# GpSimd takes three of seven taps of the second piece, and two engines' early work is reordered

## The reference

```python
w = exp(weight_gen - max(weight_gen, axis=-1))        # (4, 4096, 8, 7)
w = w / (sum(w, axis=-1) + 1e-9)
out = einsum('bshk,bskhg->bshg', w, x_unf)            # 7 taps over time, 8 heads of 24 channels
x = out.reshape(16384, 192)
h = x @ w_in                                          # 192 -> 2048
g = h * (1.0 / (1.0 + exp(-1.702 * h)))
return g @ w_out                                      # 2048 -> 192
```

## Time and profile before

| | |
|---|---|
| median of 3 runs | 1128.45 us (1128.18 to 1128.71) |
| profiled execution, its own time | 1128.58 us |
| its span, first to last instruction | 1126.8 us |
| PE busy | 1111.8 us (99%), 9748 matmuls |
| PEld busy | 914.2 us (81%) |
| DVE busy | 801.0 us (71%) |
| ACT busy | 622.1 us (55%) |
| POOL busy | 10.5 us (1%), 11 instructions |
| chain that ended last | PE 97%, ACT 1%, DVE 1% |
| granted TensorE clock | 0.999 of full speed |

### The profile page before, as it was taken

One profiled execution on the slowest core, in us unless ns is written; L12 is line 12 of the kernel. 1 busy time (PEld: TensorE's weight loads), 2 busy tenths in 40 slices (PEclk: granted clock), 3 DMA queues, 4 the chain that ended last, 5 costly groups with the idle time before them and its releaser, 6 DMA issues.

```text
span 1126.8 us, 21690 instructions
## 1 busy us (share of the span) xinstructions
PE 1111.8 (99%) x9748; PEld 914.2 (81%) x9748; DVE 801.0 (71%) x709; ACT 622.1 (55%) x659; POOL 10.5 (1%) x11
## 2 busy tenths in 40 slices
PE   6999999999999999999999999999999999999998
PEld 4788888888888888888888888888888888888886
DVE  7999988587685866859668496785957768586322
ACT  6767655555544656455464555645555555454543
POOL 2000000000000000000000000000000000000000
PEclk9999999999999999999999999999999999999999
DMA  8801010101001010010100101010010100100000
GB/s 274 243 10 54 15 54 1 40 29 40 29 1 40 29 40 29 1 48 21 40 29 12 57 1 40 29 40 29 1 40 29 40 29 1 40 29 1 29 1 29
DMA packets 9948, 43.46 MB, mean 39 GB/s; under 512 B 1088, under 2 KB 2368, under 8 KB 7552
## 3 DMA queue, kind: packets, MB, share of 16 engines
q1 hardware_dynamic: 8256, 40.24, 10.8%
q0 software_dynamic: 1456, 1.57, 0.9%
q10 hardware_dynamic: 144, 0.26, 0.1%
HBM read 24.77 MB, written 12.58 MB: 33 GB/s over the span
## 4 chain that ended last, share of the span: by engine, by line
PE 97%; ACT 1%; DVE 1%; DMA 0%; issue 0%; SPq 0%; DVEq 0%
PE hid L663 46%; PE acc_main L679 31%; PE acc_rest L679 20%; DMA gate<-in_x_first 0%; DVE hid L498 0%; ACT gate L318 0%; DVE prod L492 0%; ACT gate_hi L321 0%; ACT w L333 0%; ACT w L272 0%; ACT L318 0%; ACT L263 0%; ACT outs_main L362 0%; PE acc_main L630 0%; DVE hid L492 0%
## 5 line engine op out<-in xcount | busy, mean ns | idle before, releaser
L318 ACT ACTIVATE gate<-hid 128x1024 f32<-128x1024 f32 x256 | 263.0, 1027 | 482.6 <-PE hid L663 482.0
L577 DVE TENSOR_TENSOR gate_lo<-gate,gate_hi 128x1024 fp32r<-128x1024 f32 x256 | 312.8, 1222 | 261.0 <-ACT gate_hi L321 261.0
L663 PE MATMUL hid<-xt,w_hi 64*128 64x512 f32 x3072 | 431.4, 386 | 0.0
L663 PEld LDWEIGHTS hid<-xt,w_hi 64*128 64x128 f32 x3072 | 287.5, 184 | 61.8 <-ACT gate_hi L321 0.8
L679 PE MATMUL acc_main<-gate_hi,w 64*128 64x512 f32 x2048 | 315.6, 386 | 0.0
L321 ACT ACTIVATE gate_hi<-hid 128x1024 fp32r<-128x1024 f32 x256 | 261.1, 1020 | 0.0
L679 PEld LDWEIGHTS acc_main<-gate_hi,w 64*128 64x128 f32 x2048 | 191.7, 184 | 40.8 <-DVE gate_lo L577 0.5
L663 PE MATMUL hid<-xt,w_lo 64*128 64x512 f32 x1536 | 215.9, 386 | 0.6 <-ACT w_lo L344 0.6
L679 PE MATMUL acc_main<-gate_lo,w 64*128 64x512 f32 x1024 | 199.4, 386 | 0.0
L679 PE MATMUL acc_rest<-gate_hi,w 64*128 64x512 f32 x1024 | 199.4, 386 | 0.0
L679 PE MATMUL acc_rest<-gate_lo,w 64*128 64x512 f32 x1024 | 199.3, 386 | 0.0
(11 more groups left out here) (59 smaller groups left out, 227.4 us busy)
## 6 DMA issues: line engine op xcount, KB each, us to landing
xwin<-in_x_runs SPq DMA_DIRECT2D x15, 1056.0 KB, 4.9
out<-outs_main SPq DMA_DIRECT2D x13, 512.0 KB, 2.6
out<-outs_rest SPq DMA_DIRECT2D x13, 256.0 KB, 2.9
taps<-in_tap_runs SPq DMA_DIRECT2D x1, 3136.0 KB, 13.7
taps<-in_w_rows SPq DMA_DIRECT2D x2, 1536.0 KB, 10.0
w_hi<-w_hi SPq DMA_DIRECT2D x2, 768.0 KB, 9.5
w_lo<-w_lo SPq DMA_DIRECT2D x2, 768.0 KB, 8.0
out<-outs_main SPq DMA_DIRECT2D x5, 256.0 KB, 2.1
```

The source lines that it names most:

```text
L318: nc.scalar.activation(gate[:, v % 2, :, :], hid[:, v % 2, :, :], ACT.Gelu_apprx_sigmoid).then_inc(gate_ready, 1)
L577: nc.vector.tensor_tensor(gate_lo[:, v % SLOTS, :, :], gate[:, v % 2, :, :], gate_hi[:, v % SLOTS, :, :], ALU.subtract).then_inc(gate_lo_r ...
L663: last = nc.tensor.matmul(hid[:, v % 2, h, :], w[rows, k if j else slice_of(h, k), q, f], xt[rows, j % 2, part, k, :], start=(i == 0), sto ...
```

## The change

VectorE prepares piece 1 with four taps of its own (`own_taps`, 4 multiplications and 3 additions). The other three taps go to GpSimd: `help_with(1)`, the last entry of GpSimd's stream, behind its DMA issues L605 and L608, multiplies them from `xwin` and `tap_norm` into the unused upper halves of `prod` and `conv` (`shared_part`) and adds the three products into one. VectorE adds that one to its own sum in a new step ("help", which waits for the semaphore `helped`). Piece 1 thus has 8 tap steps on VectorE in place of 13, and the first row of `STEPS_AT` takes 15 steps in place of 20. It also takes none after unit 0, and the transposition moves from unit 6 to unit 7. On ScalarE, after unit 2, the rounding of `w1_lo` comes ahead of the negation of `w2`. Other pieces keep their steps.

```diff
@@ -23,7 +23,7 @@
 NEG_AT, ADDED_AT = 2, 5
 MAX_AT, EXP_AT = 2, 3
 
-STEPS_AT = ((2, 2, 4, 2, 4, 2, 2, 2),
+STEPS_AT = ((0, 3, 3, 2, 2, 1, 1, 3),
             (3, 4, 4, 2, 4, 6, 0, 5),
             (1, 2, 0, 6, 3, 4, 1, 2),
             (0, 2, 1, 2, 2, 1, 4, 1),
@@ -33,6 +33,8 @@
 MIXED = (2, 3, 4)
 CROSS_HI_AT, CROSS_LO_AT = (7, 7, 5), (7, 7, 5)
 WARM_UP = 4
+HELPED = (1,)
+HELP_OPS = 5
 SHARED = 3
 
 
@@ -185,6 +187,10 @@
 
         def last_cols(h):
             return slice(2 * LANES * START[LAST] + h * N, 2 * LANES * START[LAST] + (h + 1) * N)
+
+        def shared_part(j, i):
+
+            return (prod[:, 0, N_FIRST:N_CONV], prod[:, 1, N_FIRST:N_CONV], conv[:, N_FIRST:N_CONV])[i]
 
         def own(j, part):
 
@@ -327,6 +333,10 @@
                     if n == 1:
                         exponentials(1)
                         exponentials(2)
+                    if n in (2, 4):
+                        at = slice((n + 2) * P, (n + 4) * P)
+                        act.wait_ge(w1_added, 16)
+                        nc.scalar.activation(w1_lo[:, :, 0, at], w1_raw[:, :, at], ACT.Copy).then_inc(w1_late_ready, 1)
                     if n == NEG_AT:
 
                         act.wait_ge(w2_hi_ready, 3)
@@ -338,10 +348,6 @@
                         for to, of in ((MAIN_LO, MAIN), (REST_LO, REST_HI)):
                             nc.scalar.activation(w2_of(SOON, CH // 2, to), w2_of(SOON, CH // 2, of, w2_raw), ACT.Copy
                                                  ).then_inc(w2_late_ready, 1)
-                    if n in (2, 4):
-                        at = slice((n + 2) * P, (n + 4) * P)
-                        act.wait_ge(w1_added, 16)
-                        nc.scalar.activation(w1_lo[:, :, 0, at], w1_raw[:, :, at], ACT.Copy).then_inc(w1_late_ready, 1)
                     if v == EXP_AT and 1 <= j <= LAST - 2:
                         exponentials(j + 2)
                     if v == ROUND_AT[kind(j)] and j < LAST:
@@ -364,21 +370,35 @@
             act.dma_start(out[0:P, last_cols(1)], outs_main[:, 1, :]).then_inc(main_stored, 16)
 
         SOFTMAX_STEPS = 4
-        ORDER = [("mul", 0), ("mul", 1)]
-        for k in range(2, K):
-            ORDER += [("mul", k), ("add", k - 1)]
-        ORDER += [("add", K - 1)]
-        CONV_STEPS = SOFTMAX_STEPS + len(ORDER)
-        STEPS = CONV_STEPS + 2
-
-        STREAM = [(1, q) for q in range(STEPS)] + [(2, q) for q in range(STEPS - 1)]
+
+        def own_taps(j):
+
+            return ALONE if j in HELPED else K
+
+        def order(j):
+            steps = [("mul", 0), ("mul", 1)]
+            for k in range(2, own_taps(j)):
+                steps += [("mul", k), ("add", k - 1)]
+            return steps + [("add", own_taps(j) - 1)] + ([("help", 0)] if j in HELPED else [])
+
+        def conv_steps(j):
+            return SOFTMAX_STEPS + len(order(j))
+
+        def steps(j):
+
+            return conv_steps(j) + 2
+
+
+        BASE = [sum(conv_steps(i) - 1 for i in range(1, j)) for j in range(LAST + 1)]
...
         def conv_step(dve, j, q):
-            base = (j - 1) * (CONV_STEPS - 1)
+            base = BASE[j]
...
-                what, k = ORDER[q - SOFTMAX_STEPS]
+                what, k = order(j)[q - SOFTMAX_STEPS]
...
+                elif what == "help":
+                    dve.wait_ge(conv_op, base + q)
+                    dve.wait_ge(helped, HELP_OPS * (1 + HELPED.index(j)))
+                    nc.vector.tensor_tensor(acc, acc, shared_part(j, 0), ALU.add).then_inc(conv_ready, 1)
                 else:
                     last = k == K - 1
-                    dve.wait_ge(conv_op, base + q - (not last))
+                    dve.wait_ge(conv_op, base + q - (k < own_taps(j) - 1))
                     nc.vector.tensor_tensor(acc, acc, prod[:, k % 2, 0:u * CB], ALU.add
                                             ).then_inc(conv_ready if last else conv_op, 1)
 
@@ -601,6 +625,34 @@
                                         norm[:, :, i:i + 1].broadcast_to([P, g, GRP]), ALU.mult).then_inc(shared_op, 1)
             pool.wait_ge(shared_op, SHARED)
             nc.gpsimd.tensor_tensor(shared_prod[2], shared_prod[1], shared_prod[2], ALU.add).then_inc(shared_op, 1)
+            def help_with(j):
+                u = PIECES[j]
+                norm = tap_norm[:, 0:u * HB * K].rearrange("p (g k) -> p g k", k=K)
+                done = HELP_OPS * HELPED.index(j)
+
+                def mul(k, to):
+                    at = k + (NARROW if j == 3 else 0)
+                    nc.gpsimd.tensor_tensor(to.rearrange("p (g c) -> p g c", c=GRP),
+                                            xwin[:, at:at + u, :].rearrange("p t (h c) -> p (t h) c", c=GRP),
+                                            norm[:, :, k:k + 1].broadcast_to([P, u * HB, GRP]), ALU.mult
+                                            ).then_inc(helped, 1)
+
+                def add(i, value):
+                    pool.wait_ge(helped, done + value)
+                    nc.gpsimd.tensor_tensor(shared_part(j, 0), shared_part(j, 0), shared_part(j, i), ALU.add
+                                            ).then_inc(helped, 1)
+
+                pool.wait_ge(conv_op, BASE[j] + SOFTMAX_STEPS)
+                if j == 1:
+                    pool.wait_ge(x_added, 16)
+                    pool.wait_ge(head_summed, SLICES)
+                else:
+                    pool.wait_ge(x_reloaded, 16 * max(j - 2, 1))
+                for i in range(SHARED):
+                    mul(ALONE + i, shared_part(j, i))
+                for i in range(1, SHARED):
+                    add(i, SHARED + i - 1)
+
             pool.wait_ge(w1_negated, 1)
             pool.dma_start(w1_raw[:, :, LATE], w1_lo[:, :, 0, LATE].bitcast(F32), accum_op=ALU.add).then_inc(w1_added, 16)
             pool.wait_ge(w2_negated, 1)
@@ -608,6 +660,8 @@
                 pool.dma_start(w2_of(SOON, CH // 2, slice(0, D), w2_raw)[:, q],
                                w2_of(SOON, CH // 2, slice(D, 2 * D)).bitcast(F32)[:, q], accum_op=ALU.add
                                ).then_inc(w2_added, 16)
+            for j in HELPED:
+                help_with(j)
 
         @block.tensor
         def _(pe):
```

More of the change, by code:

```diff
@@ L136, in ffn_of_dynamic_conv @@
         taps_maxed, taps_shifted, taps_exped = sem("taps_maxed"), sem("taps_shifted"), sem("taps_exped")
-        conv_op, conv_ready = sem("conv_op"), sem("conv_ready")
+        conv_op, conv_ready, helped = sem("conv_op"), sem("conv_ready"), sem("helped")
         turned_ready = sem("turned_ready")
@@ L366, in ffn_of_dynamic_conv @@
         SOFTMAX_STEPS = 4
-        ORDER = [("mul", 0), ("mul", 1)]
-        for k in range(2, K):
-            ORDER += [("mul", k), ("add", k - 1)]
-        ORDER += [("add", K - 1)]
-        CONV_STEPS = SOFTMAX_STEPS + len(ORDER)
-        STEPS = CONV_STEPS + 2
-        STREAM = [(1, q) for q in range(STEPS)] + [(2, q) for q in range(STEPS - 1)]
+        def own_taps(j):
[10 more added lines that the diff above has]
+        BASE = [sum(conv_steps(i) - 1 for i in range(1, j)) for j in range(LAST + 1)]
+        STREAM = [(1, q) for q in range(steps(1))] + [(2, q) for q in range(steps(2) - 1)]
         for j in range(3, LAST + 1):
-            STREAM += [(j, q) for q in range(SOFTMAX_STEPS)] + [(j - 1, STEPS - 1)]
-            STREAM += [(j, q) for q in range(SOFTMAX_STEPS, STEPS - 1)]
-        STREAM += [(LAST, STEPS - 1)]
+            STREAM += [(j, q) for q in range(SOFTMAX_STEPS)] + [(j - 1, steps(j - 1) - 1)]
+            STREAM += [(j, q) for q in range(SOFTMAX_STEPS, steps(j) - 1)]
+        STREAM += [(LAST, steps(LAST) - 1)]
         def conv_step(dve, j, q):
-            base = (j - 1) * (CONV_STEPS - 1)
+            base = BASE[j]
             u = PIECES[j]
@@ L459, in prepare @@
                 for j, q in STREAM[first:last]:
-                    if q < CONV_STEPS:
+                    if q < conv_steps(j):
                         conv_step(dve, j, q)
-                    elif q == CONV_STEPS:
+                    elif q == conv_steps(j):
                         turn_piece(j)
```

## The result

The changed kernel takes 1136.26 us (1135.63 to 1137.09, 4 runs) against 1128.45: ratio 1.0069, 95% interval 1.0057 to 1.0081, 7.8 us slower. The profiled execution took 1135.95 us with a span of 1134.2. Forecast were 1132.2 and a range up to 1133.4. The direction was right, and so was the cause (the two engines run in turn). The size was half of what came, the time lies outside the range, and it was lost at another place than the one forecast.

What follows compares the result with a forecast made beforehand. TensorE's waits before unit 10, 2.3 us in all, bounded the gain. Other parts (+0.1) and VectorE and GpSimd in turn (+3.6) gave +3.7 us, hence 1132.2 us; range 1128.0 to 1133.4.

Steps and rivals of the forecast that it cites:

- The bound of the gain: TensorE ahead of unit 10: all waits there are together 2.3 us, so the change can give at most that.
- the sum of the other parts: Both reorderings and the later transposition, without any slowing by GpSimd: gains given back before unit 8's activation, +0.1 us in total.
- the forecast wait: ScalarE's old L339 waits for w2's DMA, landing at 39.6; unit 4's second product starts at 41.3, though 40.4 was possible.
- VectorE and GpSimd in turn: Between 34.7 and the transposition, both reading SBUF operands, the engines run in turn: transposition at 52.6 in place of 49.0.
- the upper end: Of the bounds 0 and +3.6 to +4.4 us for GpSimd's help, the one where the engines run in turn; chance 0.57.
- A: Rival: no mutual slowing of VectorE and GpSimd, help ready at 42.6, total +0.1, 1128.5 us; chance 0.22.
- B: Rival: VectorE and GpSimd overlap in part, costing between 0 and +3.6 us, 1128.5 to 1132; chance 0.13.
- C: Rival: the reorderings pay, unit 7 starts near 42.7 with no slowing by GpSimd, 0.8 us lower, 1127.6; chance 0.08.
- It can begin when L608 is issued: 31.8 + 2.6 = 34.4.: GpSimd's multiplications for piece 1 start only behind its DMA issues, at 34.4 us.
- That sum hardly depends on who goes first.: VectorE's 9.8 us plus GpSimd's 8.1 from 34.7 put the transposition near 52.6 whichever engine goes first.
- one variant (+4.4): GpSimd's three multiplications go through in a row, putting the transposition at 53.4 in place of 49.0.
- the forecast's first variant: VectorE goes first, GpSimd gets in at 41.2, VectorE waits for `helped` until 50.5; transposition at 52.6.

Runs made afterwards that it cites:

- e3: Kernel before with both reorderings (ScalarE's exchange, VectorE's first-unit steps), VectorE doing all seven taps, transposition as before; 1128.25 us, ratio 0.9999.
- e4: Changed kernel without GpSimd's five operations, three taps left out, VectorE's help step waiting for nothing; 1128.46 us, ratio 1.0002.
- e12: Changed kernel with GpSimd's five operations replaced by ten copies, each reading one SBUF operand; 1137.34 us, ratio 1.0078.
- e8: Changed kernel with GpSimd's five operations replaced by ten that only write the same areas; 1128.46 us, ratio 1.0001.
- e9: Kernel before with VectorE's taps for piece 0 in SBUF in place of PSUM; 1134.22 us, ratio 1.0052.
- e5: Changed kernel with GpSimd's operations unchanged, but VectorE does not wait for them and adds another part instead; 1136.20 us, ratio 1.0070.
- e11: Changed kernel with a 32-element GpSimd write behind its DMA issues and a wait for it ahead of the three multiplications; 1131.36 us, ratio 1.0026.
- e6: Changed kernel with GpSimd waiting for unit 3's gate_lo before its multiplications; 1131.31 us, ratio 1.0029.
- e7: Changed kernel with GpSimd waiting for its own previous multiplication before each of the next two; 1134.10 us, ratio 1.0054.

## Why the prediction was right and wrong

- *The bound of the gain, and the sum of the other parts.* Right. Unit 5 came 1.23 ahead (forecast 1.2), w2's DMA took it (e3, e4), the transposition behind unit 7 took the rest (forecast 49.0; 48.75 in e4, an execution 0.3 earlier at unit 3), and the total of +0.1 was +0.16. That the totals agree to 0.1 is luck, since neither can be told from nothing; the parts are what the rows confirm. In the changed kernel itself L349 starts at 43.99 and does not wait for the DMA: the forecast wait lies inside TensorE's 6.3 us.
- *VectorE and GpSimd in turn.* Right. The rows of before had left it open, and the upper end was a choice. It is now shown from four sides: beside GpSimd reading two operands or one, a VectorE instruction takes 6.90 or 9.06 us (after, e12); beside its writing, 0.95 and 1.22 (e8); with VectorE's taps in PSUM two L492 take 1.81, with them in SBUF 4.47 (before, e9); and the 6.90 stays where no wait for the result is involved (e5). Rivals A and B are refuted by the durations (in e11 a VectorE instruction takes 2.31, about its own 0.95 and one of GpSimd's 1.5, not a middle value), C by e4, where the DMA takes the gain. Single instructions in turn are shown in e9 (2.31 for the first L492), e6 (2.30 for an L446) and e11 (2.31 for an L435). They are not where three multiplications (6.90) or nine copies (9.06) go as one turn. Nor, as far as the rows' starts can be trusted, does the row that starts first always go first: the L435 whose row began 0.48 before GpSimd's is the one that is held (after, and alike in e5 and e7).
- *"It can begin when L608 is issued: 31.8 + 2.6 = 34.4."* Wrong, and this failed first. The issues began as forecast (31.34, with the 0.44 of this execution 31.78, against 31.8). But GpSimd's first multiplication did not wait for the end of their row: it has its own from 32.91, 1.0 us before that end, and so ahead of unit 3's `gate_lo`, which the prediction had let end at 34.7. e6 and e11, where that `gate_lo` is in time, lose 2.9 to 3.0 us instead of 7.8.
- *"That sum hardly depends on who goes first."* Wrong, and this is the step that the size hangs on. I had worked the three multiplications in a row as one variant (+4.4), but only behind unit 3's `gate_lo`. The sum adds VectorE's and GpSimd's work up to the transposition and supposes that VectorE is never idle there. In the changed kernel it was idle 2.23 ahead of unit 7's `gate_lo`, at the end of a chain through a TensorE that had lost 6.46 us at unit 3, since each unit hangs on the one before. The transposition came at 56.19 and not at 52.6, and unit 10 at 64.23 and not at 60.7 (with the 0.44, both are 4.0 late). VectorE never waited for `helped`, as the forecast's first variant had it.
- *TensorE's clock.* Left out, without a reason. Of the 7.8 us, 2.07 are one second product that took 4.34 in place of 2.27, at a granted clock of 0.51 behind the wait of 6.30. The prediction spoke of TensorE waiting and took a wait at its own length.

What the rows show of the block is this. GpSimd's first multiplication starts 1.02 us before its DMA issues' row ends in the changed kernel (32.91 against 33.93), in e5 and in e7, and e12's first copy 1.04 before (33.90 against 34.94). VectorE is then held for three multiplications in the changed kernel and in e5 (6.90), for the one that has no other right behind it in e7 (3.90), and for nine copies in e12 (9.06). In e11 the first multiplication starts 0.22 behind the end of that row (34.33 against 34.11), with the small write and the wait for it ahead of it, in e6 0.73 behind it (35.08 against 34.35), with a wait for VectorE ahead of it, and in e9 no issue runs beside the multiplications (they start at 5.93, VectorE's first L492 at 5.96, and L605 is issued at 14.31); there VectorE's turns are single ones. No run tells the DMA issue beside the first multiplication, the missing wait ahead of it and its earlier start from each other, and none shows why VectorE gets no turn within the block.

## What to carry to other kernels

Work moved to GpSimd beside VectorE was not free time here, where both read SBUF and VectorE had two operands there (in e11 five VectorE instructions of 0.95 to 1.22 us took 2.3 to 2.6): in a kernel like this count it as VectorE's own, or try a VectorE operand in PSUM, with which two multiplications took 1.81 us beside GpSimd instead of 4.47 (before, e9). Then ask at which instruction of VectorE the first turn falls, and who waits for that one: a sum of VectorE's work holds only while TensorE is not held up on the way (here it lost 6.46 us at unit 3, and VectorE later stood idle for 2.23). In e11 one small write of GpSimd and a wait for it, ahead of its multiplications, were worth 4.9 of 7.8 us. A step that takes away a wait should be followed to the next thing in line before its gain is booked; here that was a DMA that hung on the step which had been moved back.

## What was not expected of the hardware

- GpSimd instructions whose rows start before the row of its DMA issues ends held VectorE off as one block: three multiplications for 6.90 us (after, e5), nine copies for 9.06 (e12). Behind a small write and a wait for it the same multiplications and VectorE's instructions went one by one (e11, 2.3 us for what takes 0.95 alone).
- TensorE's granted clock behind a wait: 0.51 over the 4.3 us behind a wait of 6.3 us, 0.56 behind one of 4.86 (e9), 0.60 behind one of 3.05 (e7), 1.00 behind 1.51 (e11). Behind a wait of 2.19 in e6 the clock fell late: 1.00 from 48.0 to 49.0, 0.50 from 49.0 to 50.4, 0.68 from 50.4 to 53.5, 1.00 from there:

```profile
48.65 0.40 PE L734 MATMUL acc_main<-gate_lo,w 64*128 64x512 f32 x2
...
50.48 0.63 PE L734 MATMUL acc_main<-gate_lo,w 64*128 64x512 f32 x2
...
52.53 0.39 PE L734 MATMUL acc_main<-gate_lo,w 64*128 64x512 f32 x2
```

The execution of these rows took 1132.63. Three of e6's seven took 1132.1 to 1132.6 with a granted clock of 0.997 to 0.998 over the whole span, the other four 1131.1 to 1131.3 with 0.999 or more. So the same wait seems to cost the clock in some executions, about 1 us, and not in others; the one trace shows only the first kind. One of e11's ten looks alike (1132.60, 0.997). The expectation of a clock near 1.00 from 35 to 60 did not hold in it, and e6's median stands for the executions without the loss.
